# An fp32 attention and two mixers on one core: kv in float32 with K's features stationary, `out` feature-major in fp32r halves, one step table per engine

## What is computed

```python
def phi(x):
    proj = np.einsum('bhsd,df->bhsf', x, w_phi)
    proj = proj - np.max(np.abs(proj), axis=-1, keepdims=True)
    return np.concatenate([np.exp(proj), np.exp(-proj)], axis=-1)
q_p, k_p = (phi(q), phi(k))
kv = np.einsum('bhsf,bhsd->bhfd', k_p, v)
z = np.sum(k_p, axis=2)
num = np.einsum('bhsf,bhfd->bhsd', q_p, kv)
den = np.einsum('bhsf,bhf->bhs', q_p, z)[..., None] + 1e-06
```

## Time and profile before

| | |
|---|---|
| time, median of 3 runs | 1025.85 us (1024.42 to 1026.05) |
| the profiled execution | 1024.73 us |
| its span, first to last instruction | 1022.9 us |
| TensorE busy | 996.4 us (97%), 5608 matmul records |
| VectorE, ScalarE, POOL busy | 470.2, 337.3, 246.9 us |
| mean granted TensorE clock | 0.990 |

### The profile page before, as it was taken

How to read it: one execution, slowest core, us unless ns; L and a number is a source line. 1 busy time by engine, 2 the same in 40 slices (tenths; PEclk the granted TensorE clock), 3 DMA queues, 4 the chain that set the end, 5 groups by cost and what they waited for, 6 DMA issues and landing times.

```text
span 1022.9 us, 14197 instructions
## 1 busy us (share of the span) xinstructions
PE 996.4 (97%) x5608; PEld 860.8 (84%) x5608; DVE 470.2 (46%) x890; ACT 337.3 (33%) x603; POOL 246.9 (24%) x144
## 2 busy tenths in 40 slices
PE   6989899999999999999999999999999999999998
PEld 5878788888888887888888888998888888888898
DVE  5745466655576545557533333242332333342232
ACT  4654455543454424445422201341211111211111
POOL 3444564632434403443302000441000000000000
PEclk9999799999999999899999999999999999999999
DMA  8742111111212102121021001511011001001010
GB/s 226 220 163 72 47 54 46 53 46 61 66 46 65 54 19 68 53 66 46 20 69 69 1 1 45 201 64 47 0 42 46 1 28 60 1 1 42 1 42 22
DMA packets 28897, 58.13 MB, mean 57 GB/s; under 512 B 4512, under 2 KB 15008, under 8 KB 28320
## 3 DMA queue, kind: packets, MB, share of 16 engines
q1 hardware_dynamic: 20464, 47.89, 15.1%
q10 hardware_dynamic: 8368, 9.34, 2.7%
HBM read 47.78 MB, written 9.44 MB: 56 GB/s over the span
## 4 chain that ended last, share of the span: by engine, by line
PE 91%; DVE 2%; POOL 2%; DMA 2%; ACT 2%; issue 2%; SPq 0%; ACTq 0%; POOLq 0%; DVEq 0%
PE ps_ring L689 64%; PE ps_m L598 6%; PE ps_m L582 2%; PE ps_ring L598 2%; PE ps_m L615 1%; PE ps_t L552 1%; PE ps_m L509 1%; PE ps_m L510 1%; PE ps_m L508 1%; POOL k_features_lo L1059 1%; DMA kq_raw<-in_k_t 1%; PE ps_a L612 1%; PE ps_a L649 1%; PE ps_ring L509 1%; PE ps_ring L510 1%
## 5 line engine op out<-in xcount | busy, mean ns | idle before, releaser
L689 PE MATMUL ps_ring<-u_hi,w_hi 128*128 128x512 f32 (+1 forms) x560 | 212.3, 379 | 1.3 <-DVE u_full L933 1.2
L689 PE MATMUL ps_ring<-h_hi,w_hi 128*128 128x512 f32 (+1 forms) x560 | 210.7, 376 | 2.1 <-DVE u_full L933 2.1
L689 PE MATMUL ps_ring<-u_lo,w_hi 128*128 128x512 f32 (+1 forms) x560 | 207.6, 371 | 0.0
L689 PE MATMUL ps_ring<-u_hi,w_lo 128*128 128x512 f32 (+1 forms) x560 | 207.5, 371 | 0.0
L689 PE MATMUL ps_ring<-h_lo,w_hi 128*128 128x512 f32 (+1 forms) x560 | 207.1, 370 | 0.0
L689 PE MATMUL ps_ring<-h_hi,w_lo 128*128 128x512 f32 (+1 forms) x560 | 206.9, 370 | 0.0
L815 ACT ACTIVATE h_hi<-ps_ring 128x512 fp32r<-128x512 f32 (+1 forms) x140 | 77.5, 554 | 385.6 <-PE ps_ring L689 384.4
L1012 DVE SCALAR_TENSOR_TENSOR h_lo<-ps_ring,h_hi 128x512 fp32r<-128x512 f32 (+1 forms) x140 | 89.0, 637 | 221.3 <-ACT h_hi L815 221.2
L689 PEld LDWEIGHTS ps_ring<-u_hi,w_hi 128*128 128x128 f32 x560 | 106.5, 190 | 18.7 <-DVE u_full L933 1.5
L689 PEld LDWEIGHTS ps_ring<-u_hi,w_lo 128*128 128x128 f32 x560 | 106.2, 190 | 18.7
L689 PEld LDWEIGHTS ps_ring<-h_hi,w_hi 128*128 128x128 f32 x560 | 106.0, 189 | 18.6 <-DVE u_full L933 2.9
(11 more groups left out here) (147 smaller groups left out, 1251.9 us busy)
## 6 DMA issues: line engine op xcount, KB each, us to landing
...
```

The source lines that it names most:

```text
L689: last = pe.matmul(ps, w, x, start=(k, m) == (0, 0), stop=ended)
```

## The change

1. `kv` is float32 in all heads, with 128 features of K stationary and 128 columns moving: 64 columns of ones (written once, by POOL) and 64 of v. 10 matmuls, over 5 tiles of tokens for each half of the features. Its result has the features on the partitions, so that `kv_turn`, `KVT`, `round_k`, `split_v` and their tensors are gone. v is loaded without its column of ones, as 5 runs of 64 numbers in each partition.
2. `out` of steady heads is turned over: kv stationary (128 columns: 64 equal rows of denominators and 64 of x come out), 288 tokens of Q's features moving, in fp32r halves, 12 matmuls. ScalarE therefore makes Q's features twice (rounded and not), POOL takes the lo half (`QPL`), ScalarE rounds kv and VectorE takes its lo half (`KVL`). VectorE inverts the denominators through 32 x 32 transposes and writes x, features on the partitions, into `UT`. In the prologue `out` stays as it was.
3. `pair` of steady heads is cut in two: `pair_t` (transposes of `UT`), a copy by ScalarE, and `pair_u` a part later.
4. Each engine has a step table of its own (`HEAD_STEPS`, `PAIR_STEPS`) with a new `STEP_ORDER`, all chunks begin their heads at the same parts, the quarters of `mix` stand at 27, 45, 51 and 61, and the prologue has one list for each engine, in which a head's projections are followed by `out` of the head before and then its own `kv`.
5. `less_max` reads 64 partitions instead of 128.

```diff
-HEADS_AT = [[7, 13, 19, 25, 31, 37, 43, 49]] + [[5, 11, 17, 23, 29, 35, 41, 47]] * 2
-OFFSETS = {"proj_k": 0, "proj_k_last": 1, "exp_k": 1, "proj_qt": 1, "round_k": 2, "turn_r": 4, "split_v": 4, "less_max": 6, "kv": 7,
-           "kv_turn": 8, "out": 9}
-MIX_AT = [[27, 39, 51, 61], [25, 37, 49, 61], [25, 37, 49, 61]]
+HEADS_AT = [[7, 13, 19, 25, 31, 37, 43, 49], [7, 13, 19, 25, 31, 37, 43, 49], [7, 13, 19, 25, 31, 37, 43, 49]]
+HEAD_STEPS = {
+    "pe": {"proj_k": 0, "proj_k_last": 2, "proj_qt": 2, "turn_r": 4, "kv": 4, "less_max": 6, "out": 9},
+    "act": {"prep_k": 1, "exp_k": 2, "prep_q": 4, "kv": 5, "less_max": 7},
+    "dve": {"proj_k": 0, "proj_k_last": 1, "proj_qt": 2, "turn_r": 3, "kv": 5, "out": 9},
+    "pool": {"prep_k": 2, "prep_q": 4, "less_max": 6},
+}
+PAIR_STEPS = {
+    "pe": {"pair_t": 11, "pair_u": 12},
+    "act": {"pair_t": 11, "pair_u": 12},
+    "dve": {"pair_u": 12},
+    "pool": {},
+}
...
+MIX_AT = [[27, 45, 51, 61], [27, 45, 51, 61], [27, 45, 51, 61]]
...
+    for j in range(H):
+        pe += [("proj_k", j), ("proj_qt", j)]
...
+        if j > 0:
+            pe.append(("out", j - 1))
+        pe += [("turn_r", j), ("kv", j)]
...
+        pe.append(("less_max", j))
+        act.append(("less_max", j))
...
-            wait(sp, "kvt_done", n - 1)
-            sp.dma_start(V[:, h % 2], v_aug[b, h]).then_inc(sem[f"v_in_{h % 2}"], 16)
+            wait(sp, "kv_done", n - 1 if n <= H else n)
+            sp.dma_start(v(n)[:, :, DH:2 * DH], v_aug[b, h][:, :, 0:DH]).then_inc(sem[f"v_in_{h % 2}"], 16)
...
             elif name == "kv":
...
+                wait(pe, "kp_done", 2 * n + 2)
+                wait(pe, "kv_copied", n)
+                if not first:
+                    wait(pe, "kvl_done", steady(n) - 1)
+                    wait(pe, "xu_lo", before(("pair", "pair_u"), (name, n)))
+                if n == 0:
+                    pe.wait_ge(sem["v_ones"], 6)
                 wait(pe, f"v_in_{n % 2}", loaded(n // 2 + 1))
-                for t in range(ST):
-                    both = [x[:, t].rearrange("p a f -> p (a f)") for x in (kp(n), KPH, KPL)]
-                    if first:
-                        last = pe.matmul(kvt_ps, V[:, n % 2, t, :], both[0], start=(t == 0), stop=(t == ST - 1))
-                    else:
-                        last = mm3(kvt_ps, VH[:, t, :], VL[:, n % 2, t, :], both[1], both[2], t == 0, t == ST - 1)
-                last.then_inc(sem["kvt_done"], 1)
-            elif name == "kv_turn":
-                wait(pe, "kvt_copied", n + 1)
                 for a in range(2):
-                    last = pe.transpose(kv_ps[:, a, :], KVT[0:VC, a * DF:(a + 1) * DF], ID[0:VC, 0:VC])
+                    for t in range(ST):
+                        last = pe.matmul(kv_ps[:, a, :], kp(n)[:, t, a, :], v(n)[:, t, :], start=(t == 0), stop=(t == ST - 1))
...
+            elif name == "out":
+                wait(pe, "diff_done", H + before(("proj_k_last",), (name, n)))
+                wait(pe, "xt_copied", before(("pair", "pair_t"), (name, n)))
+                wait(pe, "x_done", n)
+                wait(pe, "qp_done", 2 * n + 2)
+                wait(pe, "kvl_done", steady(n))
+                for a in range(2):
+                    for c in range(2):
+                        cols = slice(c * CW, (c + 1) * CW)
+                        pe.matmul(x_ps[:, c, :], KVH[:, a, :], QPH[:, a, cols], start=(a == 0), stop=False)
+                        pe.matmul(x_ps[:, c, :], KVL[:, a, :], QPH[:, a, cols], start=False, stop=False)
+                for a in range(2):
+                    pe.wait_ge(sem["qpl_done"], 2 * steady(n) - 1 + a)
+                    for c in range(2):
+                        cols = slice(c * CW, (c + 1) * CW)
+                        last = pe.matmul(x_ps[:, c, :], KVH[:, a, :], QPL[:, a, cols], start=False, stop=(a == 1))
                 last.then_inc(sem["out_done"], 1)
...
+            elif name == "pair_t":
+                wait(pe, "x_done", n + 1)
+                wait(pe, "diff_done", H + before(("proj_k_last",), (name, n)))
+                for t in range(ST):
+                    k = min(P, S - t * P)
+                    last = pe.transpose(xt_banks[0:k, t * P:(t + 1) * P], UT[:, pn % DT, t * P:t * P + k], ID[:])
+                last.then_inc(sem["xt_done"], 1)
+            elif name == "pair_u":
+                wait(pe, "xt_copied", pn + 1)
+                wait(pe, "kvl_done", before(("kv",), (name, n)) - H)
+                for t in range(ST):
+                    k = min(P, S - t * P)
+                    last = pe.matmul(xu_bank(n), U4[0:k, t, :], XP[0:k, t, :], start=(t == 0), stop=(t == ST - 1))
                 last.then_inc(sem["xu_done"], 1)
...
             elif name == "kv":
-                act.wait_ge(sem["kvt_done"], n + 1)
-                wait(act, "kv_done", n)
-                act.copy(KVT[0:VC, :], kvt_ps).then_inc(sem["kvt_copied"], 1)
-            elif name == "kv_copy" or name == "kv_turn" and not first:
                 act.wait_ge(sem["kv_done"], n + 1)
                 wait(act, "out_done", n)
-                act.copy(KV[:], kv_ps).then_inc(sem["kv_copied"], 1)
+                if first:
+                    act.copy(KV[:], kv_ps[:, :, 2 * DH - VC:2 * DH]).then_inc(sem["kv_copied"], 1)
+                else:
+                    act.copy(KVH[:], kv_ps).then_inc(sem["kv_copied"], 1)
             elif name == "less_max":
                 act.wait_ge(sem["pt_done"], n + 1)
                 wait(act, "out_done", n)
                 for a, sign in enumerate((1.0, -1.0)):
+                    if not first:
+                        act.activation(QPH[:, a, :].rearrange("p (c n) -> p c n", c=2), turned_ps(n), ACT.Exp, scale=sign)
                     act.activation(QP[:, a, 0:S].rearrange("p (c n) -> p c n", c=2), turned_ps(n), ACT.Exp,
                                    scale=sign).then_inc(sem["qp_done"], 1)
...
+            elif name == "pair_t":
+                act.wait_ge(sem["xt_done"], pn + 1)
+                act.wait_ge(sem["xu_done"], pn)
+                act.copy(XP[:].rearrange("p t f -> p (t f)"), xt_banks).then_inc(sem["xt_copied"], 1)
...
+            elif name == "kv":
+                dve.wait_ge(sem["kv_copied"], n + 1)
+                dve.tensor_tensor(KVL[:], kv_ps, KVH[:].bitcast(F32), ALU.subtract).then_inc(sem["kvl_done"], 1)
...
+            elif name == "out":
+                rows, low = slice(n % 2 * DH, (n % 2 + 1) * DH), slice(DH, 2 * DH)
+                dve.wait_ge(sem["out_done"], n + 1)
+                dve.tensor_reduce(DENT[low], x_ps[0:DH].rearrange("p c (j t) -> p c j t", t=TB), AX.X, ALU.max,
+                                  apply_transpose=True).then_inc(sem["den_turned"], 1)
+                dve.wait_ge(sem["den_turned"], steady(n))
+                dve.tensor_scalar(DENT[low], DENT[low], EPS, None, ALU.add).then_inc(sem["den_done"], 1)
+                dve.wait_ge(sem["den_done"], n + 1)
+                dve.reciprocal(RDENT[low], DENT[low]).then_inc(sem["rden_done"], 1)
+                dve.wait_ge(sem["rden_done"], n + 1)
+                dve.transpose(RROWS[low].rearrange("p (j t) -> p j t", t=TB),
+                              RDENT[low].unsqueeze(2).to_broadcast([DH, NB, TB])).then_inc(sem["rden_rows"], 1)
+                dve.wait_ge(sem["rden_rows"], steady(n))
+                dve.tensor_tensor(UT[rows, pn % DT, :].rearrange("p (c n) -> p c n", c=2), x_ps[low],
+                                  RROWS[low].rearrange("p (c n) -> p c n", c=2), ALU.mult).then_inc(sem["x_done"], 1)
...
-            if name == "round_k":
+            if name == "less_max":
                 for a in range(2):
-                    pool.wait_ge(sem["kph_done"], 2 * steady(n) - 1 + a)
-                    pool.tensor_tensor(KPL[:, :, a, :], KP[:, :, a, :], KPH[:, :, a, :].bitcast(F32),
-                                       ALU.subtract).then_inc(sem["kpl_done"], 1)
-                done["kpl_done"] += 2
+                    pool.wait_ge(sem["qp_done"], 2 * n + 1 + a)
+                    pool.tensor_tensor(QPL[:, a, 0:S], QP[:, a, 0:S], QPH[:, a, :].bitcast(F32),
+                                       ALU.subtract).then_inc(sem["qpl_done"], 1)
+                done["qpl_done"] += 2
```

358 lines of the change are left out of this document (180 added, 178 removed).

## The result

The changed kernel takes 1016.84 us (median of 4 runs, 1015.71 to 1019.11), the one before took 1025.13 beside it: 0.9923 of it, with a 95% interval from 0.9901 to 0.9944. That is 8.3 us less, where 22.3 were forecast. The profiled execution took 1015.71 us, its span is 1013.8. The sign and most of the mechanism came true, the size did not. 1016.84 lies in the band that the prediction gave to rival 1 (1012 to 1022), but not by rival 1's mechanism: the stalls at the first heads are gone, as the next rows show.

The account below looks back on a forecast made before the run. TensorE, busy 97% of the span, bounds the kernel; other engines matter where they make it wait. From 1024.7 us: -6.9 - 15.5 - 3.3 + 2.3 + 1.1 = -22.3, giving 1002.4; forecast 994 to 1012 (0.63), 8 in 10: 989 to 1017.

Parts of the forecast that it names:

- rival 1: Stalls at the chunks' first heads stay in another form, so 15.5 us are not gained: 1018 us; chance 0.14.
- The first heads: First head of each chunk: waits for the `kv` copy and k_features_lo and the clock's falls go, -15.5 us.
- The four waits at the ring: TensorE's four waits of the ring for `u_full`, behind VectorE's v_lo, go: -3.3 us.
- Three waits at the last `mix`: Last quarter of `mix`, `pair_u` straight in front: ScalarE's cast and VectorE's subtraction lie bare, 3 x 0.75 = +2.3 us.
- QPL: POOL's lo half of Q's features in steady heads: ready before `out` needs it, with 2.2 us to spare, cost nothing.
- The upper end of +2.8: Loading v in runs under 512 B, taken at a factor of two: +2.8 us in the prologue.
- the +1.4 taken for the start: Loading v in rows of 64 numbers at the start: half the upper bound on the path, +1.4 us.
- Rival 3: VectorE, held up by POOL, late at every steady head: 1026 to 1040 us; chance 0.08 beyond 1027, 0.03 no change.
- the sum for TensorE's work, -6.9 us: Steady heads 8 to 31: `kv` +13.9, `kv_turn` -4.3, `out` -15.4, pairs +1.1, `turn_r` -2.2; ends -11 and 0.
- the prologue (+1.1 forecast: Heads before the steady ones: -4.6 - 1.8 + 6.1 + 1.4 = +1.1 us, between -5 and +5.
- The prediction's own sign of being wrong: Wrong if `out` often waits for POOL's lo half or VectorE, prologue clock falls, or float32 records exceed 0.112 us.
- The term "coming": New prologue costs: head 0 idle +2.5, VectorE and ScalarE before `kv` +0.2 x 7, late VectorE at heads 5, 7 +2.2: +6.1 us.

Follow-up runs that it names:

- b_out_late: The kernel before with `out` of the first head of each chunk two parts later on all engines, nothing else: 0.9932 of the kernel before, 7.0 us less.
- a_v4_first: The changed kernel with `split_v4` moved in VectorE's prologue list from behind head 3 to behind head 0: 0.9891 of the kernel before.
- a_rows_pair: The changed kernel with `less_max` and `pair_u`'s last tile on 128 partitions and `split_v4` behind head 0: 1002.91 us, 0.9808 of the kernel before.

## Why the prediction was right or wrong

**Right, with their sizes.**
- `kv`: 2.23 us (2.24), `out`: 1.57 (1.60), so +13.7 and -16.1 us in place of +13.9 and -15.4; `kv_turn` is gone with its 0.18.
- The first heads: no wait for the `kv` copy, clock 1.00 from 82 us to 530. That the clock is the larger share is shown by b_out_late. Each fall stands behind a wait, though not each wait brings one.
- The four waits at the ring are gone (-3.3). Each had stood right behind a v_lo, which is gone too; no run takes v_lo away alone.
- Three waits at the last `mix`: 2.3 us in all (2.3).
- `out` never waits for QPL, which the prediction had put at nothing.
- v in runs of 64 numbers: the median landing of such a load is 2.7 us against 2.8 before. The upper end of +2.8, beside which the prediction set the Trainium skill (DMA: Bandwidth & Descriptors, Specifications: the least transfer for the full rate is 512 B), did not come about for a 160 KB load here, nor did the +1.4 taken for the start: `less_max` of head 0 starts at 17.92 us against 18.57 before.
- Rival 3 did not occur. Its mechanism did, though where the prediction had not looked: in `split_v4`.

**Wrong, the step that failed: the sum for TensorE's work, -6.9 us, has no term for item 5 of the change.** `less_max` on 64 partitions was listed in the change and costed at nothing, without being named. It costs 0.38 us a head, 9.2 us over 24 heads with `pair_u`'s last tile, which the change also cut to 64 rows. The other terms of that sum came out at +13.7 - 4.3 - 16.1 and some -1.9 for the pairs and `turn_r`, together -8.6; with the rows it is +0.6. So TensorE has hardly less work than before, and nearly all that is gained behind the prologue comes from waits (6.4 + 3.3 + 1.1 = 10.8 us before, 2.3 + 2.0 = 4.3 after) and from the clock (8.0): 0.6 - 6.5 - 8.0 = -13.9, of -15.6 measured. The remaining 1.7 us I have not traced.

**Wrong, the prologue (+1.1 forecast, +6.5 measured).** The prediction's own sign of being wrong, a clock that falls in the prologue, came true. The term "coming" looked at what TensorE has to fill in with and at pmix, and left out `split_v4`. It had stood in a gap (1.54 us for the two subtractions at 35.96 us in the kernel before); in the new list it stands ahead of head 4's maxima beside two operations of POOL. 5.2 us by a_v4_first, nearly all of the 5.4 that are missing there. The lower clock of one `kv` is 2.1 of them. Since the +1.4 for v was not spent, the other parts of that sum came out 1.6 us too low, which I have not traced; where it had VectorE late at heads 5 and 7, TensorE waits for ScalarE's exponentials instead, 0.70 us each time.

**Wrong, small.** `pair_t` waits 2.0 us in all for `u_full` at the last head of each chunk, where VectorE has the `u_lo` steps of the next chunk to do just before. At two of the three waits one of these steps stands beside POOL and takes 1.79 us (at 218.64) and 1.93 (at 362.28), where the same forms take 0.62 and 0.68 elsewhere. It was not in the sum.

Together, against the sum of the prediction: +9.2 for the rows, +2.0 for `pair_t`, -1.7 where the other work came out better and -1.7 not traced make the 7.8 us missing behind the prologue; `split_v4` makes 5.2 of the 5.4 in it. With the rows and `split_v4` undone, a_rows_pair has a ratio of 0.9808, where 1002.4 of 1024.7 is 0.978. That it comes so near is in part luck: behind the first wide matmul it takes 920.3 us where the forecast has 944.0 - 23.4 = 920.6, but 3.1 us of waits of `pair_t` that the forecast lacks are set off by work that came out smaller.
